# Attention scores as one f32r product a head over stacked high and low parts, in an fp32-accurate mLSTM and feed-forward kernel

## The reference

```python
for t in range(S):                      # per batch and head
    m_new = maximum(f[t] + m, i[t])
    f_stab, i_stab = exp(f[t] + m - m_new), exp(i[t] - m_new)
    C = f_stab * C + i_stab * outer(v[t], k[t])      # 40 x 40
    n = f_stab * n + i_stab * k[t]
    y[t] = sigmoid(o[t]) * (C @ q[t]) / maximum(abs(n @ q[t]), 1)
h = x @ w_in;  x1 = (maximum(h, 0) + alpha * minimum(h, 0)) @ w_out
x2 = maximum(x1 @ w1, x1 @ w2, x1 @ w3) @ w_out2
```

## Time and profile before

| | |
|---|---|
| median of 3 runs | 756.58 us (755.68 to 757.09) |
| the profiled execution, its time | 756.52 us |
| its span | 754.8 us |
| attention and first layer interleaved, from the trace | to about 433 us |
| first layer alone, last block | 433 to 491 us |
| second feed-forward layer | 491 us to the end |

### The profile page before, as it was taken

The page is one execution under the profiler, slowest core; times in us unless marked ns, Lnnn a source line. Parts: engine busy times, 40 slices in busy tenths (PEclk is TensorE's granted clock), DMA queues, the critical chain, the costliest instruction groups (busy, mean ns, idle before and its releaser), DMA issues.

```text
span 754.8 us, 11652 instructions
## 1 busy us (share of the span) xinstructions
PE 744.0 (99%) x4472; PEld 658.5 (87%) x4472; DVE 465.2 (62%) x792; ACT 307.1 (41%) x646; POOL 184.9 (25%) x213
## 2 busy tenths in 40 slices
PE   9889999999999999999999999999999999999998
PEld 6889999999988888888888888888888888888887
DVE  8877788789788758875887646724342423324232
ACT  6655654653564446435643347221212112121211
POOL 6794334355244324432442000000000000000000
PEclk9999999999999999999999999999999999999999
DMA  9963232232232214221300090030201002010100
GB/s 233 289 194 114 79 105 67 85 108 67 80 111 83 75 41 135 70 82 46 101 1 1 21 296 1 0 119 1 78 0 44 34 1 76 1 36 0 36 1 35
DMA packets 30407, 55.66 MB, mean 74 GB/s; under 512 B 3176, under 2 KB 19024, under 8 KB 29968
## 3 DMA queue, kind: packets, MB, share of 16 engines
q1 hardware_dynamic: 29888, 54.49, 23.6%
q10 hardware_dynamic: 464, 0.43, 0.2%
HBM read 46.96 MB, written 7.95 MB: 73 GB/s over the span
## 4 chain that ended last, share of the span: by engine, by line
PE 87%; DVE 3%; POOL 3%; issue 2%; DMA 2%; SPq 1%; ACT 0%; POOLq 0%; DVEq 0%; ACTq 0%
PE bank L767 26%; PE bank L730 21%; PE bank L745 5%; PE bank L747 5%; PE bank L746 5%; PE bank L653 4%; PE bank L782 3%; PE bank L784 3%; PE bank L783 3%; PE bank L749 3%; PE bank L750 3%; PE bank L669 2%; PE bank L661 2%; DMA u_bcast<-u_scratch 2%; PE bank L691 1%
## 5 line engine op out<-in xcount | busy, mean ns | idle before, releaser
L730 PE MATMUL bank<-x_split,w_hi 128*128 128x512 f32 (+2 forms) x560 | 168.2, 368 | 0.0
L730 PE MATMUL bank<-x_split,w_lo 128*128 128x512 f32 (+2 forms) x336 | 120.9, 362 | 0.0
L913 ACT ACTIVATE g_full<-bank 128x512 f32<-128x512 f32 (+2 forms) x112 | 59.8, 534 | 140.6 <-PE bank L730 139.6
L730 PEld LDWEIGHTS bank<-x_split,w_hi 128*128 128x128 f32 x560 | 103.3, 190 | 12.3 <-ACT x_split L871 0.3
L1151 DVE SCALAR_TENSOR_TENSOR g_full<-g_full,beta,bank 128x512 f32<-128x512 f32 (+2 forms) x112 | 74.7, 667 | 40.4 <-ACT g_full L913 39.8
L1132 DVE TENSOR_TENSOR g_lo<-g_full,g_hi 128x512 fp32r<-128x512 f32 (+2 forms) x112 | 77.8, 694 | 28.6 <-ACT g_hi L922 27.9
L1172 DVE TENSOR_TENSOR best<-bank,first_of_max 128x512 f32<-128x512 f32 x36 | 24.9, 692 | 102.4 <-PE bank L767 76.1
L745 PE MATMUL bank<-g_hi,wproj 128*128 128x512 f32 (+2 forms) x224 | 84.5, 377 | 3.2 <-DVE g_lo L1132 3.2
L922 ACT ACTIVATE g_hi<-g_full 128x512 fp32r<-128x512 f32 (+2 forms) x112 | 63.1, 563 | 51.1 <-DVE g_full L1151 50.9
L747 PE MATMUL bank<-g_hi,wproj 128*128 128x512 f32 (+2 forms) x224 | 80.9, 361 | 0.0
L746 PE MATMUL bank<-g_lo,wproj 128*128 128x512 f32 (+2 forms) x224 | 80.6, 360 | 0.0
(11 more groups left out here) (135 smaller groups left out, 1453.3 us busy)
## 6 DMA issues: line engine op xcount, KB each, us to landing
u_bcast<-u_scratch SPq DMA_DIRECT2D x21, 512.0 KB, 4.2
kv<-in_kv SPq DMA_DIRECT2D x24, 324.0 KB, 3.0
q_t<-in_q_t SPq DMA_DIRECT2D x24, 180.0 KB
k_t<-in_k_t SPq DMA_DIRECT2D x72, 60.0 KB
out<-final SPq DMA_DIRECT2D x5, 640.0 KB, 3.8
wproj_raw<-in_w_out SPq DMA_DIRECT2D x4, 640.0 KB, 10.5
o_gate<-in_o_gate SPq DMA_DIRECT2D x4, 640.0 KB, 4.9
w_raw<-in_w_max SPq DMA_DIRECT2D x2, 1152.0 KB, 6.7
```

The costliest lines, as they stand in the source:

```text
L730: ins = pe.matmul(ps[:, 0:cols], w[:, a, f], xs[:, x, 0:cols], start=(m == 0), stop=(m == 7))
L913: act.activation(gf[:, n % GF_SLOTS, 0:cols], hid[j % HID_BANKS][:, 0:cols], ACT.Relu, scale=-1.0).then_inc(neg_done, 1)
```

## The change

From chunk 3 on, a head's scores come from one f32r product. q and k load once each into `qk` (120 rows, two slots instead of three). In a new step `stack`, placed right after `carry` of the chunk before, ACT rounds both to f32r (the high parts), DVE subtracts to get the low parts, and SP issues 9 transfers inside SBUF. They put k-high, k-low and q-high, q-low of each head on top of each other in 120 rows, in the pairs (high, low), (low, high) and (high, high): `qks`. One f32r product over these 120 rows adds the three terms high·low, low·high and high·high. The term low·low is left out. Chunks 0 to 2 are as before, with three single `k_t` buffers that share their place with `qks` and `parts`.

In SP's loop kv and u are issued first, then q and k (after a wait for the carry product two chunks back), then the 9 transfers of the chunk before. `store_rows` and `load_o` stand one chunk earlier.

```diff
+STACK = SLOTS
+TERMS = 3
@@ chunk_groups
-    return [[("scores", ch)], [("carry", ch)],
+    split = STACK <= ch + 1 < NCH
+    return [[("scores", ch)], [("carry", ch)] + split * [("stack", ch + 1)],
...
-        qt, _ = sb("q_t", [128, SLOTS, NK, L], F32)
-        kt, _ = sb("k_t", [128, SLOTS, KH * NK, L], F32)
+        qk, _ = sb("qk_t", [128, 2, 2, NK * L], F32)
+        qks, qks_at = sb("qk_stacked", [128, 2, KH * NK, L], F32R)
+        parts, parts_at = sb("qk_parts", [128, 4, NK * L], F32R)
...
+        def load_qk(eng, ch):
+            c = ch % 2
+            wait(eng, scored, NG if ch == 2 else 0)
+            wait(eng, carry_out, ch - 2)
+            eng.dma_start(qk[0:KR, c, 0, :], q_t[ch]).then_inc(qk_loaded[c], 16)
+            if ch < STACK:
...
+            else:
+                eng.dma_start(qk[0:KR, c, 1, :], k_t[ch].rearrange("a d t -> (a d) t")).then_inc(qk_loaded[c], 16)
...
+        def stack(eng, ch):
+            eng.wait_ge(scored, NG * max(ch, 2))
+            eng.wait_ge(qk_split, ch - STACK + 1)
+            for n in range(TERMS):
+                pair = (slice(1, 3), slice(1, 4, 2), slice(0, 3, 2))[n]
+                for a in range(KH):
+                    eng.dma_start(qks[n * D:(n + 1) * D, :, a * NK:(a + 1) * NK, :].rearrange("p n g t -> p n (g t)").bitcast(F32),
+                                  parts[a * D:(a + 1) * D, pair, :].bitcast(F32)).then_inc(stacked, 16)
@@ SP's loop
             for ch in range(SLOTS + 1, NCH):
-                load_chunk(sp, ch)
+                load_kv(sp, ch)
                 load_u(sp, ch)
+                load_qk(sp, ch)
+                stack(sp, ch - 1)
...
-                    if ch == min(FIRST[b + 2] + SLOTS, NCH) - 1:
+                    if ch == FIRST[b + 2] + 1:
                         store_rows(b)
...
+            stack(sp, NCH - 1)
@@ PE
-                    pe.wait_ge(qk_loaded[c], QK_LOADS * nth)
+                    if ch < STACK:
+                        pe.wait_ge(qk_loaded[ch % 2], qk_loads(ch))
+                    else:
+                        pe.wait_ge(stacked, 16 * TERMS * KH * (ch - STACK + 1))
...
+                            if ch < STACK:
+                                lhs, rhs = kt[ch][0:KR, at, :], qk[0:KR, ch % 2, 0, of * L:(of + 1) * L]
+                            else:
+                                lhs, rhs = qks[0:KR, 1, at, :], qks[0:KR, 0, at, :]
+                            ins = pe.matmul(ps[:, k * L:(k + 1) * L], lhs, rhs, start=True, stop=True)
@@ ACT
+                if kind == "stack":
+                    act.wait_ge(qk_loaded[ch % 2], qk_loads(ch))
+                    act.wait_ge(scored, NG * STACK)
+                    wait(act, stacked, 16 * TERMS * KH * (ch - STACK))
+                    act.activation(parts[0:KR, 1:3, :], qk[0:KR, ch % 2, :, :], ACT.Copy).then_inc(qk_high, 1)
@@ DVE
+                if kind == "stack":
+                    dve.wait_ge(qk_high, ch - STACK + 1)
+                    dve.tensor_tensor(parts[0:KR, 0:4:3, :], qk[0:KR, ch % 2, :, :], parts[0:KR, 1:3, :].bitcast(F32),
+                                      ALU.subtract).then_inc(qk_split, 1)
```

More of the change, by code:

```diff
@@ L158, with qk_loads @@
 W2_LOW_AT = {5: (0,), 6: (1, 2), 7: (3, 4), 8: (5, 6), 9: (7, 8), 10: (9, 10), 11: (11,)}
+def qk_loads(ch):
+    return sum(16 * (1 + KH) if n < STACK else 32 for n in range(ch % 2, ch + 1, 2))
 class Links:
@@ L235, in build @@
         end_at = cursor[0]
+        kt = [sb(f"k_t{c}", [128, KH * NK, L], F32, at)[0]
+              for c, at in enumerate((qks_at, qks_at + KH * NK * L * 4, parts_at))]
         pick, _ = sb("pick_head", [128, H, L], F32, prob_r_at)
@@ L323, in build @@
         w_split = sem("weights_split")
-        qk_loaded = [sem(f"qk_loaded{c}") for c in range(SLOTS)]
+        qk_loaded = [sem("qk_loaded_a"), sem("qk_loaded_b")]
+        qk_high = sem("qk_high")
+        qk_split = sem("qk_split")
+        stacked = sem("stacked")
         u_loaded = [sem(f"u_loaded{c}") for c in range(SLOTS)]
@@ L476, in _ @@
             sp.wait_ge(k_cleared[0], 1)
-            load_chunk(sp, 0)
+            load_qk(sp, 0)
+            load_kv(sp, 0)
             sp.wait_ge(k_cleared[1], 1)
-            load_chunk(sp, 1)
+            load_qk(sp, 1)
+            load_kv(sp, 1)
             load_w1(sp, 0, range(3))
@@ L483, in _ @@
             sp.wait_ge(k_cleared[2], 1)
-            load_chunk(sp, 2)
+            load_qk(sp, 2)
+            load_kv(sp, 2)
             load_o(sp, 1)
@@ L491, in _ @@
             load_w1(sp, 2, range(3))
-            load_chunk(sp, 3)
+            load_qk(sp, 3)
+            load_kv(sp, 3)
             sp.wait_ge(u_stored[0], 16)
@@ L651, in attention @@
                         for k in range(HG):
-                            h = g * HG + k
-                            ins = pe.matmul(ps[:, k * L:(k + 1) * L], kt[0:KR, c, h % KH * NK + h // KH, :], qt[0:KR, c, h // KH, :],
-                                            start=True, stop=True)
+                            of, n = divmod(g * HG + k, KH)
+                            at = n * NK + of
+                            if ch < STACK:
[3 more added lines that the diff above has]
+                            ins = pe.matmul(ps[:, k * L:(k + 1) * L], lhs, rhs, start=True, stop=True)
                         ins.then_inc(scored, 1)
@@ L660, in attention @@
                         o = g * KH * DE
-                        ins = pe.matmul(ps[:, g * COLS:(g + 1) * COLS], qt[0:KR, c, g, :], state[0:KR, o:o + COLS],
+                        ins = pe.matmul(ps[:, g * COLS:(g + 1) * COLS], qk[0:KR, ch % 2, 0, g * L:(g + 1) * L], state[0:KR, o:o + COLS],
                                         start=True, stop=True)
@@ L984, in _ @@
             dve.sem_inc(best_ready, CREDIT2)
-            dve.memset(kt[:, 0, :, :], 0.0).then_inc(k_cleared[0], 1)
+            dve.memset(kt[0][:, :, :], 0.0).then_inc(k_cleared[0], 1)
             dve.memset(gates[:, U, 0:ON_PE * L], 0.0)
@@ L1227, in _ @@
             pool.memset(still[:, :], 0.0).then_inc(still_set, 1)
-            pool.memset(kt[:, 1, :, :], 0.0).then_inc(k_cleared[1], 1)
+            pool.memset(kt[1][:, :, :], 0.0).then_inc(k_cleared[1], 1)
             pool.memset(ident[:, :], 0.0)
@@ L1246, in _ @@
             pool.memset(tables[:, 1, :, :], 0.0).then_inc(tables_cleared, 1)
-            pool.memset(kt[:, 2, :, :], 0.0).then_inc(k_cleared[2], 1)
+            pool.memset(kt[2][:, :, :], 0.0).then_inc(k_cleared[2], 1)
             pool.memset(state_dec[:, :], 0.0).then_inc(decayed, 1)
@@ L1358 @@
         "i_gate": i_gate.reshape(B * H, S),
-        "q_t": nine(q).transpose(0, 2, 3, 1, 4).reshape(NCH, KR, NK, L),
-        "k_t": nine(k).transpose(0, 2, 3, 1, 4),
+        "q_t": nine(q).transpose(0, 2, 3, 1, 4).reshape(NCH, KR, NK * L),
+        "k_t": nine(k).transpose(0, 2, 3, 1, 4).reshape(NCH, KH, D, NK * L),
         "kv": np.concatenate([tokens(k), tokens(np.concatenate([v, np.ones_like(v[..., :1])], axis=3))], axis=2),
```

9 lines of the change are left out of this document (4 added, 5 removed).

## The result

The changed kernel takes 791.43 us (median of four runs, 789.89 to 791.56), the kernel before beside it 756.59. The ratio is 1.0459, 95% interval 1.0442 to 1.0475: 35 us slower, where I had forecast 13 us faster. It is the rival that the stacking lands late.

The account below looks back on a forecast made before the run. PE, busy 99% of the span, was taken as the bound, with DVE nearest. Shorter products -17.9, late `project` +1.0 and waits +3.5 summed to -13.4 us, from 756.52 to 743.1 us, range 737 to 757.

Parts of the forecast that it names:

- the rival that the stacking lands late: Wait ahead of scores: nine transfers land well beyond 6.5 us, a loss from 8.4 us, 779.6 at 10; chance 0.10.
- What bounds the kernel: Whole span: PE is busy 99% and is the bound; DVE comes nearest, 54.8 busy of 62.8 us from 141 us.
- Product of 106 ns, 0.85 us saved a chunk: PE's scores, chunks 3 to 23: f32r products at 106 ns cut 1.70 to 0.85 us a chunk, saving 17.9 us.
- The rival of a short product that is no faster: PE's scores: 128-column f32r products keep fp32's 213 ns a head, nothing saved, 761.0 us; chance 0.10.
- Copy and subtraction: Per chunk, 120 x 768 each: a copy on ACT of about 0.84 us, a subtraction on DVE of about 0.95.
- the +1.0: After chunk 2's carry: subtraction stands ahead of DVE's `g_lo`, so PE starts `project` about 1.0 us later, once.
- The landing of the nine transfers: Ahead of stacked scores: all nine land 6.5 us after the first issue, taken between 5.1 and 7.8.
- The waits, 3.5 us in 5 places: PE ahead of scores of chunks 9, 10, 13, 17, 21: waits of 2.3 + 0.3 + 0.9 us for transfers.
- the rival's own rule: Late stacking: each us beyond 6.5 costs 7 us; at 10, about eight other chunks add 1.5 us each.
- DVE "fits by a hair": Stretch from 141 us: four subtractions raise DVE to 58.6 us busy, just within the shortened stretch of 59.4.
- the rival of DVE as the bound (750): From 141 to 203.8 us: subtraction takes 1.5 us beside POOL, 750; DVE or late transfers in part, chance 0.16.
- Moved steps: SP's list: kv and u ahead of q and k, `store_rows` and `load_o` one chunk earlier; lead covers it, no cost.

Follow-up runs that it names:

- e3: Changed kernel with PE's stacked scores reading ready weights without waiting, and the nine transfers a chunk and ACT's wait for them left out: 744.21 us.
- e5: Changed kernel with the nine transfers reading q from DRAM instead of SBUF, PE multiplying weights but still waiting for them: 798.53 us.
- e7: Changed kernel with four of the nine transfers issued from ACT's queue, the other five from SP's: 831.2 us.
- e12: e10 without the subtraction, the transfers carrying high parts in place of the low ones: 740.5 us.
- e10: e6 with the gates' load one chunk later still and chunk 3 left in fp32: 752.84 us, ratio 0.9951 to the kernel before.
- e1: Changed kernel with the stack step ahead of the previous chunk's scores and the nine transfers ahead of the next q and k load: 772.63 us.
- e6: e1 with the stores of rows and the gates' load one chunk later in SP's list: 756.92 us.
- e11: e10 with the subtraction of q and k done by POOL (GpSimd) instead of DVE: 761.08 us.
- e4: Changed kernel with each of the nine transfers cut in two, one for q and one for k, 18 a chunk: 895.59 us.

## Why the prediction was wrong, by its steps

**What bounds the kernel** held: PE is the bound, and DVE the next.

**Product of 106 ns, 0.85 us saved a chunk** held. The fourth to sixth blocks, four chunks each, went from 76.4 to 72.9 us in e3, 0.87 a chunk, and the eight products take 0.84 us. The rival of a short product that is no faster is out, and so are, for these products, the Trainium skill's 81 ns of TensorE: Matmul & The Clock Gate, Back-to-back issue gap: the row with 41 columns was the right one to follow.

**Copy and subtraction** took 0.84 and 0.95 us (median; 1.49 in the first chunk, beside POOL); `project` after chunk 2's carry starts at 44.64 us instead of 43.63: the +1.0 came as forecast.

**The landing of the nine transfers** is the step that failed. It was taken as 6.5 us after the first issue, with 7.8 as the upper bound, and was 9.6. "SP issues the three k transfers in 1.08 us, so 9 take 3.2 us" is the sentence: they took 7.3, since an issue with its source inside SBUF takes 0.77 to 0.82 us where one out of DRAM takes 0.35 (e5). That, with the 2.3 us after the last issue, is 9.6. The bound was no bound, as it was drawn from loads out of DRAM, where the prediction itself said that no row shows a transfer inside SBUF. The other term of that step was too small as well: it spread the packets over 16 engines, 3.3 us, where ten carry them, 5.9 us at the 82 ns measured. Quicker issues alone don't help, since this second limit lies at about the same place: 10.9 us in e5 and 9.5 in e7, each with kv and u beside. The rest of the chain held: chunk 9's wait was put at 2.3 us for a landing of 6.5, which makes 5.4 at 9.6, and 5.19 was measured. The prediction had given a stacking that is clearly late a chance of 0.10.

**The waits, 3.5 us in 5 places** were the term mis-sized by that: 31.9 us in 13, and 47.4 with all that follows. By the rival's own rule, break-even at 8.4 us and 779.6 at 10, a landing of 9.6 gives 743.1 + 7 x 3.1 + 8 x 1.1 = 773.6. The rest, up to 791, is 17.8 us. The rule left out three things of that size: the half clock behind the longer waits (at most 18.5 us), ACT's own waits for the last transfers, which start the next parts late (16.8 us, in part under PE's waits), and DVE in the third block (4.6, next paragraph). No run divides the rest among them.

**DVE "fits by a hair"** in the third block: it doesn't. e3, with no wait for transfers, took 64.0 us there instead of 62.8 less 3.4. These 4.6 us are why even e3's span falls by 12.4 us and not by the 16.9 of my terms without waits; the other blocks fell as forecast. So the rival of DVE as the bound (750) holds in part as well. e12 prices the subtraction at 12.3 us in e10's order, 4.5 of them in the third block; in the changed kernel's order it isn't priced.

**Moved steps**: store and gates' load one chunk earlier were costed at nothing for kv and u, which held. What was not costed is that they share queue and transfer engines with the nine. Moving them is worth 15.7 us between e1 and e6; in the changed kernel's order it wasn't tried.

## What to carry to other kernels

Count the transfers of a step before their bytes: price each issue from a row with the same kind of source, and the engines by the rows of its shape, and when no row has that source, make the chance of the worse case as large as the ignorance. A cheaper issue and more engines have to come together where both limits lie close. A wait of several us can cost PE more than its length, since the clock comes back late; find it a place with room on both sides, and keep bulk stores and loads away from the few microseconds in which it must land. Low parts made by the engine that is already second busiest can eat the gain of a cheaper product, and moving them to its neighbour can cost more than they did.

## What the hardware showed that I had not expected

- A transfer from SBUF to SBUF holds its issuing queue for 768 ns (706 with half the rows in it), one of the same shape from DRAM for 346. On two queues at once each still takes 0.8.
- GpSimd's 120x768 subtraction beside VectorE's 128x512 subtraction of two SBUF inputs and beside what GpSimd then runs later lengthened the latter from 862 to 1581 ns on average (e10, e11).
- A transfer of 40 rows on SP's queue adds ten packets under 512 B (e4: 1890 for 189).
- Nine SBUF to SBUF transfers of 120 KB land 9.4 to 10.0 us after the first issue from one queue, and 9.5 from two that issue them in 4.1 us.
- 189 transfers of 120 KB beside a PE at 98% took nothing from it (744.36 and 744.21 us with and without them).
- The granted clock fell to 0.50 within a gap of 5.2 us without a matmul, and was back some 4 us after PE began again.
